# The order of the three matmuls of a split product in a float32r attention and two-MLP kernel

## The chip, the cores and the metric

The kernel runs on one core of one Trainium2 chip. The metric is the device time of one execution in microseconds, and three runs were made of the kernel before: 2424.06, 2426.97 and 2427.41 us, a median of 2426.97 us. Durations below come from one profiled execution of the same kernel, whose span, from its first instruction to its last, is 2422.0 us.

## The reference

```python
# q, k, v: (2, 6016, 256) float32; tau: scalar
qn = q / (norm(q, axis=1) + 1e-6);  kn = k / (norm(k, axis=1) + 1e-6)
a = softmax(kn.transpose(0, 2, 1) @ qn / tau, axis=-1)        # 256 x 256 for each batch
x = (v @ a).reshape(12032, 256)
x = (sigmoid(x @ w_gate) * (x @ w_val)) @ w_out               # w_gate, w_val: 256 x 1536
h = x @ w2_in                                                 # w2_in: 256 x 2048
out = (h - tanh(h)) @ w2_out                                  # 12032 x 256
```

## The kernel before

Attention is over channels, so its matrix is only 256 x 256 for each of the two batches. The kernel first streams q and k in and accumulates their product in plain float32 (`gram_chunk`, line 767), and sums squares on ScalarE and VectorE beside it. It makes the softmax, turns it (`turn_att`, line 787) and folds it into the weights: `fold` multiplies the attention matrix by `w_gate` and `w_val`, 512 columns at a time, so that v can be fed to the first MLP directly. There are 12 folds, 6 for each batch.

From there on the work goes in 32 tiles of T = 376 rows of v, 16 tiles for each batch. A tile has two stages. In the first, `U(j)` multiplies the turned v by a block of 128 columns of the gate and of the val weights, for j = 0 to 11, and `D(t, j)` multiplies the gated product by a block of `w_out` into the two banks `x2_acc`. In the second, `P_(t, i)` multiplies that result by a block of 128 columns of `w2_in`, for i = 0 to 15, and `O(t, i)` multiplies h - tanh(h) by a block of `w2_out` into `acc`. TensorE works through one hand-written order (`body`): U runs three blocks ahead of D, P_ four blocks ahead of O, and some blocks of the next tile's U are mixed into the seam between the tiles. ScalarE takes sigmoid or tanh of a finished bank and rounds the product to its high half, VectorE multiplies and makes the low half. All engines are tied by counting semaphores. TensorE waits for `g_lo_made` ahead of a D or an O, for `prod_made` ahead of a U or a P_ (its bank must be free), and for `x2_lo_made` or `acc_read_dve` ahead of a tile's first P_ or U.

Apart from the gram matrix, every product is made of halves. Each float32 operand is held as two float32r tensors, `_hi` (rounded) and `_lo` (the rest), and a product is the sum of three matmuls, high by low, low by high and high by high; low by low is left out. All of these come out of the helper `product3`, whose matmul stands on line 740. `pe.matmul(psum, a, b)` has `a` as the stationary operand (128 x 128, loaded into the array) and `b` as the moving one (376 columns in U, D and P_, 256 in O, 512 in a fold). The trace writes a matmul as output<-moving,stationary, and shows for each matmul a LDWEIGHTS of its own on the row PEld. The stationary operand is the weights in U, D and P_, the activations `g2` in O, and the turned attention in a fold. In O it has 128 columns twice and then 120, since 376 rows are 128 + 128 + 120. In the trace `x_hi`/`x_lo` are the `x2` pair, `g_hi`/`g_lo` the `g1` or `g2` pair, `x_acc` the banks `x2_acc`.

A tile has 12 x 12 matmuls in U, 12 x 6 in D, 16 x 6 in P_ and 16 x 9 in O, which is 456. Over 32 tiles these are 9984 matmuls of 376 columns and 4608 of 256. The folds add 144 of 512 columns. Divided by three that is 3328, 1536 and 48 groups, 4912 in all. No wait and no semaphore stands inside a group: the callers put their waits ahead of it, and the increment is attached to the last matmul that `product3` returns.

Of the kernel before, what the change touches and what calls it, by code (L numbers as in the profile page):

```python
# [7 lines left out]
def attn_two_mlp_kernel(  # L8
# [105 lines left out]
    with ExitStack() as ctx:  # L114
# [620 lines left out]
        def _(pe):  # L735
            def product3(psum, w, x, start, stop, shared_bank=False):

                (w_hi, w_lo), (x_hi_, x_lo_) = w, x
                for n, (a, b) in enumerate(((w_hi, x_lo_), (w_lo, x_hi_), (w_hi, x_hi_))):
                    mm = pe.matmul(psum, a, b, start=start and n == 0, stop=stop and n == 2,  # L740
                                   skip_group_check=shared_bank)
                return mm
# [48 lines left out]
            def fold(b, n, psums):  # L791

                _, w_hi, w_lo = pieces[n]
                for h in range(KC):
                    for kc in range(KC):
                        mm = product3(psums[h][:, :], both(ATT_T, ALL, kc, cols(h)),
                                      (w_hi[:, kc, :], w_lo[:, kc, :]), kc == 0, kc == KC - 1)
                mm.then_inc(fold_made, 1)

            def U(j):  # L800

                for n, w in enumerate((GATE, VAL)):
                    for kc in range(KC):
                        mm = product3(up[2 * (j % 2) + n][:, 0:T], both(w, ALL, kc, cols(j % J1)),
                                      both(VT, ALL, kc, ALL), kc == 0, kc == KC - 1)
                mm.then_inc(up_made, 1)

            def D(t, j):
                pe.wait_ge(g_lo_made, t * PER_TILE + j + 1)
                for h in range(KC):  # L810
                    mm = product3(x2_acc[h][:, 0:T], both(WOUT, ALL, j, cols(h)),
                                  both(G1, ALL, j % SLOTS, ALL), j == 0, j == J1 - 1)
                    if j == J1 - 1 and h == 0:
                        mm.then_inc(x2_half_made, 1)
                mm.then_inc(down_made, 1)
# [139 lines left out]
```

## Time and profile before

| | |
|---|---|
| median of three runs | 2426.97 us (2424.06 to 2427.41) |
| span of the profiled execution | 2422.0 us |
| TensorE matmul busy | 2391.3 us, 99%, 15132 instructions |
| TensorE weight load busy | 2366.7 us, 98%, 15132 instructions |
| VectorE busy | 1205.0 us, 50% |
| ScalarE busy | 1030.4 us, 43% |
| share of `product3` (line 740) on the chain that ended last | 94% |

Matmuls are pipelined, and the recorded duration of one overlaps the next. The time that a matmul takes out of the span is therefore read from start to start of neighbouring rows in the timeline, and not from its duration. Starts are given to 0.01 us, so the interval is taken over a stretch of rows.

### The profile page before, as it was taken

The numbers are of one execution on the slowest core, as the hardware profiler recorded it, in microseconds if no ns is written. First come the engines' busy times: TensorE is split into PE (matmuls) and PEld (weight loads), VectorE is DVE, ScalarE is ACT, GpSimd is POOL, SyncE is SP. The second block draws the span as 40 slices with busy tenths as digits, with TensorE's granted clock in tenths as the row PEclk, the third lists the DMA queues.
The fourth block names the chain that finished last, engine by engine and source line by source line (L and its number), as shares of the span: only waits on it lengthen the run. The fifth ranks groups of instructions, "written<-read, shape, count | busy, mean of one in ns | idle before, by whom it ended". The sixth has DMA issues, their size and how long they took to land.

```text
span 2422.0 us, 39823 instructions
## 1 busy us (share of the span) xinstructions
PE 2391.3 (99%) x15132; PEld 2366.7 (98%) x15132; DVE 1205.0 (50%) x2115; ACT 1030.4 (43%) x2062; POOL 105.8 (4%) x76
## 2 busy tenths in 40 slices
PE   8999999999999999999999999999999999999999
PEld 6789999999999999999989999999999999999999
DVE  6874444444444444444554444544444454444444
ACT  5543444444344444434433444444344444434443
POOL 3540000000000000000120000000000000000000
PEclk9999999999999999999999999999999999999999
DMA  9620000000000000000010000000000000000000
GB/s 309 216 68 14 7 13 7 13 13 13 13 6 13 7 13 13 13 13 7 21 33 14 13 7 13 7 13 13 13 13 6 13 7 13 13 13 11 9 6 7
DMA packets 128450, 62.08 MB, mean 26 GB/s; under 512 B 104992, under 2 KB 117280, under 8 KB 128416
## 3 DMA queue, kind: packets, MB, share of 16 engines
q1 hardware_dynamic: 125104, 49.56, 7.8%
q0 software_dynamic: 3312, 12.06, 1.5%
q8 instruction: 22, 0.36, 0.1%
q14 instruction: 12, 0.10, 0.0%
HBM read 49.28 MB, written 12.32 MB: 25 GB/s over the span
## 4 chain that ended last, share of the span: by engine, by line
PE 95%; DVE 2%; issue 1%; ACT 1%; SPq 1%; DMA 1%; DVEq 0%; ACTq 0%
PE up L740 55%; PE acc L740 22%; PE x_acc L740 17%; PE x_acc L767 1%; DVE sq_sum L529 1%; DMA qk_in<-in_k 1%; DVE g_lo L644 0%; SPq L303 0%; DVE vt_lo L621 0%; ACT squares L391 0%; SPq L287 0%; DVE norm L562 0%; DVE product L635 0%; ACT g_hi L442 0%; DVE norm L567 0%
## 5 line engine op out<-in xcount | busy, mean ns | idle before, releaser
L434 ACT ACTIVATE func_out<-up 128x376 f32<-128x376 f32 x896 | 433.5, 484 | 679.6 <-PE up L740 664.6
L644 DVE TENSOR_TENSOR g_lo<-product,g_hi 128x376 fp32r<-128x376 f32 x896 | 502.5, 561 | 433.8 <-ACT g_hi L442 429.6
L442 ACT ACTIVATE g_hi<-product 128x376 fp32r<-128x376 f32 x896 | 463.0, 517 | 491.9 <-DVE product L638 266.1
L635 DVE TENSOR_TENSOR product<-up,func_out 128x376 f32<-128x376 f32 x384 | 210.7, 549 | 485.3 <-ACT func_out L434 485.2
L740 PE MATMUL acc<-out_w_hi,g_lo 128*128 128x256 f32 (+1 forms) x1536 | 431.2, 281 | 0.0
L740 PE MATMUL acc<-out_w_lo,g_hi 128*128 128x256 f32 (+1 forms) x1536 | 430.5, 280 | 0.0
L740 PE MATMUL acc<-out_w_hi,g_hi 128*128 128x256 f32 (+1 forms) x1536 | 430.1, 280 | 0.0
L638 DVE TENSOR_TENSOR product<-up,func_out 128x376 f32<-128x376 f32 x512 | 280.8, 548 | 138.4 <-ACT func_out L434 126.0
L740 PE MATMUL up<-x_lo,in_w_hi 128*128 128x376 f32 x1024 | 341.6, 334 | 1.0 <-DVE x_lo L627 1.0
L740 PE MATMUL up<-x_hi,in_w_hi 128*128 128x376 f32 x1024 | 341.2, 333 | 0.0
L740 PE MATMUL up<-x_hi,in_w_lo 128*128 128x376 f32 x1024 | 340.0, 332 | 0.0
L740 PEld LDWEIGHTS acc<-out_w_hi,g_lo 128*128 128x128 f32 (+1 forms) x1536 | 286.0, 186 | 0.0
L740 PEld LDWEIGHTS acc<-out_w_lo,g_hi 128*128 128x128 f32 (+1 forms) x1536 | 285.8, 186 | 0.0
L740 PEld LDWEIGHTS acc<-out_w_hi,g_hi 128*128 128x128 f32 (+1 forms) x1536 | 285.7, 186 | 0.0
L740 PE MATMUL up<-vt_lo,gate_w_hi 128*128 128x376 f32 x768 | 257.0, 335 | 6.0 <-DVE product L635 3.9
L740 PE MATMUL x_acc<-g_lo,out_w_hi 128*128 128x376 f32 x768 | 257.5, 335 | 5.1 <-DVE g_lo L644 5.1
L740 PE MATMUL up<-vt_hi,gate_w_hi 128*128 128x376 f32 x768 | 257.5, 335 | 0.0
L740 PE MATMUL x_acc<-g_hi,out_w_hi 128*128 128x376 f32 x768 | 257.5, 335 | 0.0
L740 PE MATMUL up<-vt_hi,val_w_hi 128*128 128x376 f32 x768 | 257.1, 335 | 0.0
L740 PE MATMUL up<-vt_hi,gate_w_lo 128*128 128x376 f32 x768 | 256.8, 334 | 0.0
L740 PE MATMUL up<-vt_hi,val_w_lo 128*128 128x376 f32 x768 | 256.6, 334 | 0.0
L740 PE MATMUL x_acc<-g_hi,out_w_lo 128*128 128x376 f32 x768 | 256.4, 334 | 0.0
(111 smaller groups left out, 2899.9 us busy)
## 6 DMA issues: line engine op xcount, KB each, us to landing
v_in<-in_v SPq DMA_DIRECT2D x248, 48.0 KB, 2.0
qk_in<-in_q SPq DMA_DIRECT2D x29, 384.0 KB, 4.2
qk_in<-in_k SPq DMA_DIRECT2D x29, 384.0 KB, 5.3
out_rows<-out_sb SPq DMA_DIRECT2D x32, 256.0 KB, 2.2
out_rows<-out_sb SPq DMA_DIRECT2D x32, 120.0 KB, 2.2
w_stage<-in_moe_w_out POOLq DMA_DIRECT2D x7, 512.0 KB, 4.2
w_stage<-in_moe_w_gate POOLq DMA_DIRECT2D x6, 512.0 KB, 4.3
w_stage<-in_moe_w_val POOLq DMA_DIRECT2D x6, 512.0 KB, 5.4
```

The source lines that it names most:

```text
L434: act.activation(func_out[:, half, :], src[:, 0:T], func).then_inc(func_made, 1)
L442: act.activation(hi[:, i % SLOTS, :], product[:, half, :], ACT.Copy).then_inc(g_hi_made, 1)
L529: dve.tensor_tensor(sq_sum[:, which, 0:size, :], sq_sum[:, which, 0:size, :], squares[:, which, 0:size, :], ALU.add).then_inc(sq_added, 1)
L635: dve.tensor_tensor(product[:, half, :], up[2 * (i % 2) + 1][:, 0:T], func_out[:, half, :], ALU.mult).then_inc(prod_made, 1)
L638: dve.tensor_tensor(product[:, half, :], up[i % 4][:, 0:T], func_out[:, half, :], ALU.subtract).then_inc(prod_made, 1)
L644: dve.tensor_tensor(lo[:, i % SLOTS, :], product[:, half, :], hi[:, i % SLOTS, :].bitcast(F32), ALU.subtract).then_inc(g_lo_made, 1)
L740: mm = pe.matmul(psum, a, b, start=start and n == 0, stop=stop and n == 2, skip_group_check=shared_bank)
L767: mm = pe.matmul(gram[b][:, h * C:(h + 1) * C], qk_in[:, buf, 1, s, cols(h)], qk_in[:, buf, 0, s, :], start=first and s == 0 and h == 0, s ...
```

## The change

The three matmuls of a group are issued in another order. Before they were (high stationary, low moving), (low, high), (high, high); after they are (low stationary, high moving), (high, high), (high, low). The flags that open and close an accumulation stay with the first and the last of the group.

```diff
@@ -736,7 +736,7 @@
             def product3(psum, w, x, start, stop, shared_bank=False):
 
                 (w_hi, w_lo), (x_hi_, x_lo_) = w, x
-                for n, (a, b) in enumerate(((w_hi, x_lo_), (w_lo, x_hi_), (w_hi, x_hi_))):
+                for n, (a, b) in enumerate(((w_lo, x_hi_), (w_hi, x_hi_), (w_hi, x_lo_))):
                     mm = pe.matmul(psum, a, b, start=start and n == 0, stop=stop and n == 2,
                                    skip_group_check=shared_bank)
                 return mm
```

## Rows read from the trace of the kernel before

**Rows 1.** The page: busy time, share of the span and instructions of each engine
```profile
PE 2391.3 (99%) x15132; PEld 2366.7 (98%) x15132; DVE 1205.0 (50%) x2115; ACT 1030.4 (43%) x2062; POOL 105.8 (4%) x76
```

**Rows 2.** The page: chain that ended last, share of the span by engine
```profile
PE 95%; DVE 2%; issue 1%; ACT 1%; SPq 1%; DMA 1%; DVEq 0%; ACTq 0%
```

**Rows 3.** The waits of PE: who waited for whom, us in total, times, longest
```profile
PE x_acc L767 <- DMA qk_in<-in_k: 9.6, 7, 3.5
PE x_acc L740 <- DVE g_lo L644: 5.1, 1, 5.1
PE up L740 <- DVE product L635: 3.9, 2, 3.4
```

**Rows 4.** Stretches of the span: length, busy us (instructions) of each engine, clock, DMA, GB/s
```profile
400.00:800.00 400.00, 400.00 (x2590) 400.00 (x2590) 186.67 (x346) 166.14 (x340) 0.00 (x0) 1.00 0.05 11
```

**Rows 5.** Timeline of U and D: start us, us, engine, line, operation, out<-moving,stationary
```profile
1299.99 0.34 PE L740 MATMUL x_acc<-g_hi,out_w_hi 128*128 128x376 f32 x1
...
1303.09 0.33 PE L740 MATMUL x_acc<-g_hi,out_w_hi 128*128 128x376 f32 x1
```

**Rows 6.** Timeline of P_, then of O, stationary of 128 and of 120 columns
```profile
249.70 0.34 PE L740 MATMUL up<-x_lo,in_w_hi 128*128 128x376 f32 x1
...
251.24 0.28 PE L740 MATMUL acc<-out_w_lo,g_hi 128*128 128x256 f32 x1
...
251.94 0.28 PE L740 MATMUL acc<-out_w_lo,g_hi 128*120 128x256 f32 x1
...
252.30 0.33 PE L740 MATMUL up<-x_lo,in_w_hi 128*128 128x376 f32 x1
```

**Rows 7.** Timeline of a fold, PE: first matmul after a wait, then the stream
```profile
1242.20 0.50 PE L740 MATMUL x_acc<-gate_w_lo,att_t_hi 128*128 128x512 f32 x1 [0.23 <-DVE att_t_lo L599]
1242.53 0.40 PE L740 MATMUL x_acc<-gate_w_hi,att_t_lo 128*128 128x512 f32 x1
1242.77 0.39 PE L740 MATMUL x_acc<-gate_w_hi,att_t_hi 128*128 128x512 f32 x1
...
1244.81 0.39 PE L740 MATMUL x_acc<-gate_w_hi,att_t_hi 128*128 128x512 f32 x1
```

**Rows 8.** Timeline of the same fold, weight loads alone
```profile
1242.20 0.19 PEld L740 LDWEIGHTS x_acc<-gate_w_lo,att_t_hi 128*128 128x128 f32 x1 [0.54 <-DVE att_t_lo L599]
1242.31 0.19 PEld L740 LDWEIGHTS x_acc<-gate_w_hi,att_t_lo 128*128 128x128 f32 x1
1242.54 0.19 PEld L740 LDWEIGHTS x_acc<-gate_w_hi,att_t_hi 128*128 128x128 f32 x1
```

**Rows 9.** Timeline of U, matmuls and weight loads together
```profile
1306.87 0.33 PE L740 MATMUL up<-vt_lo,gate_w_hi 128*128 128x376 f32 x1
1306.87 0.19 PEld L740 LDWEIGHTS up<-vt_hi,gate_w_lo 128*128 128x128 f32 x1
1307.04 0.34 PE L740 MATMUL up<-vt_hi,gate_w_lo 128*128 128x376 f32 x1
1307.04 0.19 PEld L740 LDWEIGHTS up<-vt_hi,gate_w_hi 128*128 128x128 f32 x1
1307.22 0.33 PE L740 MATMUL up<-vt_hi,gate_w_hi 128*128 128x376 f32 x1
```

## Prediction

> **What bounds the kernel now.** I read the busy shares first, then the chain that ended last, then what TensorE waited for, and last the timeline of each stage. TensorE is busy for 99% of the span, VectorE for half and ScalarE for 43% [rows 1]. Busy shares of a pipelined engine overlap, so the chain decides, and it runs through TensorE for 95% of the span [rows 2]. TensorE's own waits are few: the longest entries are 9.6 us for the loads of q and k, 5.1 us once for a low half of g and 3.9 us for two products [rows 3]. Between 400 and 800 us the matmul row has no gap at all, the granted clock is 1.00, the 2.4 GHz level, and VectorE is busy for 187 of 400 us [rows 4]. So the time is the number of matmuls by their interval, and no other engine is near. Whatever the change brings, it brings through the interval of the 14736 matmuls of `product3`, or it brings nothing.
>
> **The intervals.** In U and D 18 intervals lie between the first and the last row shown: (1303.09 - 1299.99) / 18 = 172.2 ns [rows 5]. In P_ nine intervals of 376 columns take 251.24 - 249.70 = 1.54 us, 171.1 ns each; in O nine intervals of 256 columns take 252.30 - 251.24 = 1.06 us, 117.8 ns each [rows 6]. In a fold nine intervals of 512 columns take 1244.81 - 1242.77 = 2.04 us, 226.7 ns each [rows 7]. At 2.4 GHz, one column a cycle, the columns alone would take 156.7, 106.7 and 213.3 ns. What is over is 15.5 ns in U and D, 14.4 in P_, 11.1 in O and 13.3 in a fold: a nearly fixed cost for each pair of load and matmul. The sum over `product3` is 6912 x 172.2 + 3072 x 171.1 + 4608 x 117.8 + 144 x 226.7 ns = 1190.2 + 525.6 + 542.8 + 32.6 = 2291.2 us of the span of 2422.0 us. The other 130.8 us are the float32 gram matrix, the softmax and the waits, and the change touches none of them.
>
> **The change, part by part.** It removes no instruction that the source names and adds none. Each of the 4912 groups has the same three matmuls with the same columns. No wait stands inside a group, and the callers wait for the low half ahead of the whole group, so nothing can start sooner because the low moving operand is now used last; those edits cost nothing, and the 5.1 and 3.9 us of waits [rows 3] stay where they are. The increment stays on the third matmul, so the readers ScalarE and VectorE get the bank at the same time as before, if the three intervals together are the same. SP's and POOL's queues are not passed by anything.
>
> What is new is that the third matmul needs the stationary operand that the second one has. Whether its LDWEIGHTS goes away is the whole question, and the trace of before can't show it: nowhere in it do two neighbours have the same stationary operand. What it does show is one load for each matmul, 15132 of both [rows 1], as the helper calls `matmul` each time and nothing in the change tells it to leave a load out. I take it that the load stays, 15132 after as before. The source asks for it with every call, and no row shows a load left out.
>
> If the load stays, what is it worth that its content is already in the array? Loads lie beside work: the load for the next matmul starts in the moment in which the running one starts, 1306.87 and 1307.04 us [rows 9]. Its own length can be read where nothing covers it, at the start of a fold: the next load starts 0.11 us after the first [rows 8]. Both 172 ns and 117.8 ns cover 110 ns. Nor does a shorter load shorten the interval: with 120 stationary columns three matmuls of O take 252.30 - 251.94 = 0.36 us, 120 ns each, against 0.70 us / 6 = 116.7 ns with 128 [rows 6]. So the length of the load is hidden, and only a fixed cost of exchanging the operand, if it is part of the 11 to 15 ns, is on the path. An engine that carries out the load pays that cost, whatever was in the array. I take 0, between -68 us (worked out below, all of it gone) and +11 us, the operand bound below.
>
> **The order itself.** The same shape costs 172.2 ns in U and D and 171.1 ns in P_ [rows 5, 6]. The two differ in their tiles and banks, so placement of operands is worth about 1.1 ns. After the change the pairs of operand streamed and operand loaded beside it are the same kinds as before: before, low beside low, high beside high, and high beside the next group's high; after, high beside high twice, and low beside the next group's low. I see no reason for a sign and take 0; the bound is 9984 x 1.1 ns = 11 us to either side.
>
> The sum: the span stays at 2422.0 us. The runs' median lies 5.0 us over the profiled span, from outside the span and from spread, and that stays too. Forecast 2427 us.
>
> **A rule beside the trace.** A load takes 110 ns here and starts with the matmul ahead of it [rows 8, 9]. The Trainium skill, "TensorE: Matmul & The Clock Gate", section "LDWEIGHTS (loading the stationary operand)", gives its columns over 1.2 GHz, an estimate of 107 ns, and the trace agrees. The same page, under "Step-by-step: what each phase is for", says that loads are pulled ahead of matmuls in flight if they go to a background buffer, and that is the rule that speaks against a gain here: by it the sum stays at 2427 us. Its section "Back-to-back issue gap" gives an isolated matmul N/2.4 + 2.5 ns, 159.2 ns for 376 columns; no row here shows a matmul without a load. By that rule, if the third load were gone, one in three of the intervals would fall by 13.0, 11.9, 8.6 and 10.8 ns, 2304 x 13.0 + 1024 x 11.9 + 1536 x 8.6 + 48 x 10.8 = 56 us, an estimate of 2371 us.
>
> **Rival 1: the repeated load is left out,** by whatever turns the program into instructions or by the engine. For it speaks that every interval has 11 to 15 ns over its columns, at three sizes. Against it, that the trace has exactly as many loads as matmuls. Its price at most is the whole excess for one matmul in three: 2304 x 15.5 + 1024 x 14.4 + 1536 x 11.1 + 48 x 13.3 ns = 35.7 + 14.7 + 17.0 + 0.6 = 68 us, so 2359 us; if only half of the excess belongs to the load, 2393 us. VectorE's half share leaves room for it [rows 4]. Chance 0.10.
>
> **Rival 2: a load of the operand that is in use is not hidden.** It ends on the slow side. The place is between the second and the third matmul of a group: the load of the high half repeats what the running matmul works with, and could be held until that one has gone through. The price of an uncovered load is read at the start of a fold, where matmul two follows matmul one after 0.33 us, against 227 ns in the stream: about 100 ns [rows 7]. Fully uncovered it gives 4912 x 0.1 = 491 us, 2918 us. It decides from 1 ns a group on, 4.9 us or 0.2%. Against it: the moving operand is already the same for two neighbours, the high half in the second and third matmul, and shows no stall [rows 9]. A repeated moving operand says little of a repeated stationary one, though. Chance 0.02.
>
> **Rival 3: the order moves the interval a little.** Mechanism and price as worked out above: up to 1.1 ns on the 9984 matmuls of 376 columns, 2416 to 2438 us; it decides from 0.5 ns on. What speaks for it is that two stages of one shape differ; against it, that the kinds of pairs are the same. Chance 0.05 on the fast side beyond 0.2% and 0.07 on the slow side, the latter more because the seam between groups now has the low load of the next group beside it, with a new bank at times.
>
> **How the numbers follow.** The forecast, no change beyond 0.2%, gets what is left: 0.76. About 0.2% (4.9 us) is what a measurement of this kernel can tell from no change; the three runs of before span 3.4 us. Faster: 0.10 + 0.05 = 0.15. Slower: 0.02 + 0.07 = 0.09. The range takes in the forecast and rival 3 on both sides, 0.88 together, and leaves out rivals 1 and 2, 0.12. With the 11 us bound and the spread of the runs it is 2414 to 2439 us.
>
> **What would show it.** Count loads first: 15132 if I am right, 15132 - 4912 = 10220 if rival 1 holds by way of the program. Then the intervals of U, P_, O and a fold again: 172, 171, 118 and 227 ns by the forecast; by rival 1 the third start of a group would be followed, or preceded, by an interval near 157 ns; by rival 2 the interval from the second to the third matmul would be long, up to 270 ns. With equal counts but intervals down by some ns, the engine would find the exchange of an equal operand cheaper, and my step from a hidden load to no gain would be the wrong one. If the medians differ by over 0.2% with all intervals the same, the difference would have to lie in the waits [rows 3].

## The result and the profile after

The changed kernel takes 2433.59 us, the median of seven runs (2431.28 to 2435.59); beside them the kernel before took 2427.14 us, also the median of seven (2424.06 to 2430.48). The ratio is 1.0027, with a 95% interval from 1.0017 to 1.0038. It is slower by 0.27%, 6.5 us, a little more than the 0.2% that was taken as the limit of what can be told.

The page of the kernel after, its busy times, to be read beside [rows 1]:

```profile
span 2431.8 us, 39823 instructions
## 1 busy us (share of the span) xinstructions
PE 2394.9 (98%) x15132; PEld 2371.7 (98%) x15132; DVE 1208.0 (50%) x2115; ACT 1030.4 (42%) x2062; POOL 104.3 (4%) x76
...
## 4 chain that ended last, share of the span: by engine, by line
PE 94%; DVE 2%; issue 1%; DMA 1%; ACT 1%; SPq 0%; ACTq 0%; DVEq 0%
```

All 15132 loads are still there, and the chain runs through TensorE as in [rows 2]. The repeated load lies beside the running matmul like any other. Here is a group of P_ in which that can be seen:

```profile
249.93 0.33 PE L740 MATMUL up<-x_hi,in_w_lo 128*128 128x376 f32 x1
...
250.10 0.33 PE L740 MATMUL up<-x_hi,in_w_hi 128*128 128x376 f32 x1
250.10 0.19 PEld L740 LDWEIGHTS up<-x_lo,in_w_hi 128*128 128x128 f32 x1
250.27 0.34 PE L740 MATMUL up<-x_lo,in_w_hi 128*128 128x376 f32 x1
```

The second and the third matmul both have `in_w_hi` as the stationary operand. The third one's load starts at 250.10 us with the second matmul, and the third matmul follows 0.17 us later. The waits of PE after, the longest of them, in the columns of [rows 3]:

```profile
PE acc L776 <- DVE expd L549: 11.3, 1, 11.3
PE x_acc L767 <- DMA qk_in<-in_k: 7.5, 6, 3.8
PE x_acc L740 <- DVE g_lo L644: 5.1, 1, 5.1
PE up L740 <- DVE product L635: 3.9, 2, 3.4
```

Waits of `product3` are as before, 5.1 and 3.9 us. The 11.3 us are a wait that ends at 65 us, in the head of the kernel, ahead of the first fold, so before any matmul of `product3`; it is 3.0 to 12.9 us long in the kernels of this study, 3.7 us in the kernel before. The stretch of [rows 4] after:

```profile
400.00:800.00 400.00, 400.00 (x2590) 400.00 (x2589) 186.47 (x346) 166.53 (x341) 0.00 (x0) 1.00 0.05 11
```

No gap, the same clock. A window cut at round numbers is too coarse for 0.3%: it holds 2590 matmuls again, because it starts at another point of the tile. What shows it is the length of a tile, read from the same matmul in different tiles. The first matmul of P_ in the second and in the fourteenth tile, 12 tiles apart, in the timeline of the kernel before:

```profile
246.11 0.33 PE L740 MATMUL up<-x_lo,in_w_hi 128*128 128x376 f32 x1
...
1092.75 0.33 PE L740 MATMUL up<-x_lo,in_w_hi 128*128 128x376 f32 x1
```

and in that of the kernel after:

```profile
249.93 0.33 PE L740 MATMUL up<-x_hi,in_w_lo 128*128 128x376 f32 x1
...
255.11 0.28 PE L740 MATMUL acc<-out_w_hi,g_lo 128*128 128x256 f32 x1
...
1098.88 0.33 PE L740 MATMUL up<-x_hi,in_w_lo 128*128 128x376 f32 x1
```

A tile took 846.64 / 12 = 70.55 us and takes 848.95 / 12 = 70.75 us, 0.19 us more. Usual tiles of one execution (all but the last and the two at the change of batch) differ from one another by 0.01 us at most, the rounding of the starts, so this number is far sharper than the time of a run. Times 32 tiles it is 6.2 us, all but 0.3 us of the 6.5 us between the medians. The profiled spans differ by 9.8 us; of this 3.6 us lie before the first P_ matmul of the kernel (175.56 and 179.18 us), in the head. They are there before the new order has done anything. This is the first matmul of the first fold, which is the first of `product3`, before and then after:

```profile
95.05 0.50 PE L740 MATMUL up<-gate_w_lo,att_t_hi 128*128 128x512 f32 x1 [1.01 <-DVE att_t_lo L599]
```

```profile
98.92 0.50 PE L740 MATMUL up<-gate_w_hi,att_t_lo 128*128 128x512 f32 x1 [1.02 <-DVE att_t_lo L599]
```

No matmul in the new order comes before these. From there to the first matmul of U (125.96 and 129.84 us) it is 30.9 us in both, so the stretch of the folds is as long as before. The head's 3.6 us arise in a part of the kernel that the change doesn't touch. That part varies: the first fold starts between 93.81 and 100.35 us in the profiles of this study.

The stages inside the tile, as the mean interval from one start to the next over all matmuls of a stage in the trace (intervals over 1.2 times the usual one left out, some 3060 of P_ and 2290 to 4607 of the others kept), in ns:

| stage | before | after | difference | matmuls a tile |
|---|---|---|---|---|
| U | 172.2 | 171.7 | -0.5 | 144 |
| D | 172.0 | 171.4 | -0.7 | 72 |
| P_ | 170.9 | 172.9 | +2.1 | 96 |
| O | 117.9 | 118.6 | +0.7 | 144 |

With unrounded values 96 x 2.07 + 144 x 0.67 - 144 x 0.45 - 72 x 0.68 ns = 0.18 us of the 0.19. P_ adds 0.20 us and O 0.10 us to a tile, and U and D give 0.11 us of it back. In the rows above, the first 30 intervals of P_ take 255.11 - 249.93 = 5.18 us, where before 251.24 [rows 6] - 246.11 = 5.13 us. So it is one instruction stream with all counts equal, and its stages move by small amounts of either sign.

A stage's mean hides more than it shows. Number the 456 matmuls of a usual tile by their place in it, and take the mean interval at each place over 27 tiles of the trace before: at 376 columns these go from 165 to 178 ns, at 256 columns from 112 to 125 ns, and at every place all 27 tiles agree to 1 ns. It is no noise but a fixed pattern, and the new order is another pattern.

### The profile page after: what moved, and what is told of

Its sections match the earlier page's. It is cut to its first block, busy times and chain, and to the rows that moved or that the text cites. A ratio compares the mean times of both kernels' runs of the same rounds, so it can differ in the third digit from the quotient of the medians.

```text
span 2431.8 us, 39823 instructions
## 1 busy us (share of the span) xinstructions
PE 2394.9 (98%) x15132; PEld 2371.7 (98%) x15132; DVE 1208.0 (50%) x2115; ACT 1030.4 (42%) x2062; POOL 104.3 (4%) x76
## 4 chain that ended last, share of the span: by engine, by line
PE 94%; DVE 2%; issue 1%; DMA 1%; ACT 1%; SPq 0%; ACTq 0%; DVEq 0%
PE up L740 55%; PE acc L740 22%; PE x_acc L740 17%; DMA qk_in<-in_k 1%; PE x_acc L767 1%; DVE sq_sum L529 1%; DVE g_lo L644 0%; ACT squares L391 0%; DVE vt_lo L621 0%; SPq L287 0%; DVE norm L562 0%; DVE product L635 0%; ACT g_hi L442 0%; DVE norm L567 0%; DVE norm L566 0%
## 5 line engine op out<-in xcount | busy, mean ns | idle before, releaser
L740 PE MATMUL up<-vt_lo,val_w_hi 128*128 128x376 f32 x768 | 256.7, 334 | 0.0
```

## The experiments

Four accounts were held against each other: that the order sets the interval of a stage through the addresses of what is streamed and loaded (called the theory of place below); that a repeated stationary operand is worth something; that TensorE meets ScalarE and VectorE in memory; and that the values in the array count. The helper was given a stage name, so that the order could be chosen for each stage:

```diff
-            def product3(psum, w, x, start, stop, shared_bank=False):
+            ORDER = {'P': ('LH', 'HH', 'HL')}
+            def product3(psum, w, x, start, stop, shared_bank=False, stage="F"):
...
-                for n, (a, b) in enumerate(((w_hi, x_lo_), (w_lo, x_hi_), (w_hi, x_hi_))):
+                pairs = {"HL": (w_hi, x_lo_), "LH": (w_lo, x_hi_), "HH": (w_hi, x_hi_)}
+                for n, (a, b) in enumerate(pairs[name] for name in ORDER.get(stage, ('HL', 'LH', 'HH'))):
```

Names give the stationary half first: HL is high stationary by low moving. The order of before is HL LH HH, the changed one LH HH HL. The diffs of the orders are against the kernel before.

Only P_ alone, U and D alone, and the order by stage were run often enough (8 to 12 executions) to compare times. The others ran once: 2426.77 and 2428.54 us with x2 moved (old and new order), 2424.40 us with x2 moved by a multiple of 2048, 2426.42 us with ScalarE later, 2421.23 us with the zeros, and 2427.16 (HH HL LH), 2427.80 (HL HH LH), 2427.43 (LH HL HH) and 2427.85 us (HH LH HL). The kernel before took 2425.52 and 2428.71 us in single executions beside them. These times tell nothing at this size; what is read from these experiments is the tile, start to start.

**The new order in P_ alone** (the diff above).

> The new order in P_ alone, all other stages as before. Both profiles repeat to 0.01 us from tile to tile: 70.55 us before, 70.75 us after, and between starts of neighbouring matmuls P_ went from 170.9 to 172.9 ns, U from 172.2 to 171.7, D from 172.0 to 171.3, O from 117.8 to 118.4. Theory (the order sets the interval of each stage by itself): P_ near 172.9 ns, the others as before, a usual tile of 70.75 us, about 6 us over before, ratio 1.002 to 1.003. Rival (the interval of a stage hangs on what its neighbours do, or the change of a whole tile has one cause that the order in P_ alone does not carry): P_ stays near 170.9 ns, the tile near 70.55 us, ratio 1.000. Rival that the difference comes from the head of the kernel: ratio 1.000, since the folds are as before.

Measured: 2429.97 us against 2425.43 us, ratio 1.0020 (1.0010 to 1.0029). The same two matmuls, 12 tiles apart:

```profile
248.14 0.33 PE L743 MATMUL up<-x_hi,in_w_lo 128*128 128x376 f32 x1
...
1096.22 0.33 PE L743 MATMUL up<-x_hi,in_w_lo 128*128 128x376 f32 x1
```

A tile of 70.67 us. P_ took 172.6 ns, U 172.2 and D 172.0 as before. The tile fell short of the 70.75 us expected, since P_ rose by 1.7 and not by 2.1 ns, and since O, whose order was not touched, fell from 117.9 to 117.6 ns. P_ and O alternate in the stream, and what stands beside a matmul counts too. The new order in P_ alone costs 0.12 us a tile, part of the 0.19.

**The new order in U and D alone.**

```diff
+            ORDER = {'U': ('LH', 'HH', 'HL'), 'D': ('LH', 'HH', 'HL')}
```

> The new order in U and D alone; P_, O and the folds as before. Theory (each stage by itself): U near 171.7 and D near 171.3 ns, so a tile gains 144 x 0.45 + 72 x 0.7 ns = 0.11 us, 70.44 us, about 3.6 us in all, ratio 0.9985, faster than both kernels. Rival (intervals hang on the neighbours or on chance of the execution): U and D as before at 172.2 and 172.0 ns, ratio 1.000 or above.

Measured: 2422.80 us against 2425.43 us, ratio 0.9987 (0.9979 to 0.9996). Twelve tiles:

```profile
245.46 0.33 PE L743 MATMUL up<-x_lo,in_w_hi 128*128 128x376 f32 x1
...
1090.50 0.33 PE L743 MATMUL up<-x_lo,in_w_hi 128*128 128x376 f32 x1
```

70.42 us a tile, 0.13 less than before; U 171.7, D 171.1, P_ 170.9, O 117.9 ns. As expected, this part of the change is a small gain.

The two runs together say something about O. The new order in P_ adds 0.12 us a tile and in U and D it takes 0.13 us off, so these three stages alone would leave the tile as it was. Yet the changed kernel's tile is 0.19 us longer. The other 0.2 us, about 6.6 us in 32 tiles and as much as the whole measured loss, come only when O has the new order beside them: O goes from 117.6 ns with the order changed in P_ alone to 118.6 ns, P_ from 172.6 to 172.9 ns. The new order in O alone was not run, so how much of this is O's own and how much its meeting with P_ stays open.

**x2 at another address, old order.** P_ streams x2. It was moved behind all other tensors, and a dummy holds its old place:

```diff
-        x2_hi, x2_lo = pair("x2", [P, KC, T])
+        x2_gap = sb("x2_gap", [P, 2, KC, T])
...
         out_sb = sb("out_sb", [P, len(SUBS), C])
+        x2_pad = sb("x2_pad", [P, 72])
+        x2_hi, x2_lo = pair("x2", [P, KC, T])
```

> The order of before, with the two halves of x2, which P_ streams, at another place of SBUF (45472 bytes a partition further on, 416 beyond a multiple of 2048). No other tensor moves. Theory of place (the interval depends on where the streamed and the loaded operand lie): P_ moves away from 170.9 ns by more than 0.3 ns, in either direction, and U and O stay at 172.2 and 117.8. Rival (values in the array, or the order as such): P_ stays within 0.2 ns of 170.9, tile 70.55 us.

```profile
243.77 0.34 PE L742 MATMUL up<-x_lo,in_w_hi 128*128 128x376 f32 x1
...
248.93 0.28 PE L742 MATMUL acc<-out_w_lo,g_hi 128*128 128x256 f32 x1
...
1092.41 0.34 PE L742 MATMUL up<-x_lo,in_w_hi 128*128 128x376 f32 x1
```

A tile of 70.72 us, almost what the changed order costs, with nothing changed in the order. P_ went to 171.7 ns, U stayed near its 172.2 (172.3) and D at 172.0. O was expected to stay at 117.8 and went to 118.3: again the neighbour of P_ moved with it.

**x2 at that other address, new order.** The same diff on the changed kernel.

> The new order everywhere, with x2 at the same other place as in the run before this one. Theory of place: P_ moves away from 172.9 ns, and the difference between the two orders in P_, 2.1 ns at the old place, is another one here, perhaps of the other sign. Rival (the order as such costs 2.1 ns in P_): P_ stays 2.1 ns over the run with the old order at this place.

```profile
249.00 0.34 PE L742 MATMUL up<-x_hi,in_w_lo 128*128 128x376 f32 x1
...
254.14 0.28 PE L742 MATMUL acc<-out_w_hi,g_lo 128*128 128x256 f32 x1
...
1096.36 0.34 PE L742 MATMUL up<-x_hi,in_w_lo 128*128 128x376 f32 x1
```

70.61 us a tile, P_ at 171.5 ns. At this address the new order is the better one, by 0.11 us a tile, and P_ costs 0.2 ns less with it instead of 2.1 more. U and D gain as they did at the old address, and O is slower by 0.4 ns. The first 30 intervals of P_ take 5.14 us here and 5.16 with the old order, against 5.18 and 5.13 at the old address. The loss of the changed kernel is not a property of the order; it is the order together with where the tensors lie.

**x2 moved by a multiple of 2048 bytes, old order.** The output rows' tensor and a dummy fill the old place.

```diff
-        x2_hi, x2_lo = pair("x2", [P, KC, T])
+        out_sb = sb("out_sb", [P, len(SUBS), C])
+        x2_gap = sb("x2_gap", [P, 736])
...
-        out_sb = sb("out_sb", [P, len(SUBS), C])
+        x2_pad = sb("x2_pad", [P, 224])
+        x2_hi, x2_lo = pair("x2", [P, KC, T])
```

> The order of before, with x2 moved by 43008 bytes a partition, 21 times 2048, where the earlier move was 22 times 2048 and 416 more. The tensor of the output rows, which TensorE doesn't touch, takes part of the old place; nothing else moves. In both traces the intervals of U and P_ inside a tile repeat with every fourth block of 128 weight columns, that is every 2048 bytes. Theory (the address counts by its remainder to 2048): P_ 170.9 ns and a tile of 70.55 us, as before. Rival (any other address changes it, or a coarser bank than 2048 bytes counts): P_ moves by 0.3 ns or more and the tile leaves 70.55 us by more than 0.03.

```profile
245.70 0.33 PE L742 MATMUL up<-x_lo,in_w_hi 128*128 128x376 f32 x1
...
1092.34 0.33 PE L742 MATMUL up<-x_lo,in_w_hi 128*128 128x376 f32 x1
```

846.64 us for 12 tiles, to the last digit as before, and each of the 456 places of a tile has its old interval to within 0.1 ns. A move about as long as the one above, with remainder 0 instead of 416 bytes, changes nothing. So it is not the move that counts; the two moves fit the remainder of the address to 2048 bytes, or to a divisor of it. No third address was tried.

**ScalarE's and VectorE's work later, old order.**

```diff
...
+                if not isinstance(n, int) or n > 1:
+                    act.wait_ge(extra_made, n - 1)
+                act.activation(extra[:, :], src[:, 0:T], func).then_inc(extra_made, 1)
                 act.activation(func_out[:, half, :], src[:, 0:T], func).then_inc(func_made, 1)
```

> The order of before. ScalarE applies sigmoid or tanh to each finished bank twice, the first time into a tensor that nothing reads, so that everything ScalarE and VectorE do in the tiles comes about 0.48 us later against TensorE's matmuls, and there is half as much again for ScalarE to do. No operand of TensorE moves. Theory (the interval is set by TensorE's own two reads, streamed operand and loaded operand, by where they lie): U 172.2, D 172.0, P_ 170.9, O 117.8 ns and a tile of 70.55 us, as before. Rival (the intervals come from TensorE's meeting with ScalarE and VectorE in SBUF or PSUM): they move by 0.3 ns or more, the tile by 0.1 us or more.

The page's busy times and the twelve tiles:

```profile
PE 2389.7 (99%) x15132; PEld 2365.6 (98%) x15132; DVE 1211.1 (50%) x2115; ACT 1330.4 (55%) x2958; POOL 105.1 (4%) x76
```

```profile
247.51 0.33 PE L746 MATMUL up<-x_lo,in_w_hi 128*128 128x376 f32 x1
...
1094.15 0.33 PE L746 MATMUL up<-x_lo,in_w_hi 128*128 128x376 f32 x1
```

846.64 us again, with 300 us more of ScalarE. That is less than the half as much again that was expected, and the shift is not an even 0.48 us either: in a usual tile, the products come 0.4 us later in most places and up to 1.2 us in some, the halves of vt hardly at all. Even so, each of the 456 places has its old interval to within 0.1 ns. Had TensorE's meeting with the others in memory set the pattern, it would have moved where they moved; it is ruled out as the cause.

**Zeros in the array.** The low half of `w2_in` is made as high minus high.

```diff
-                pool.tensor_tensor(lo, staged(n), hi.bitcast(F32), ALU.subtract).then_inc(w_split, 1)
+                rest_of = hi.bitcast(F32) if SECOND_BLOCK <= n < SECOND_BLOCK + 2 * J2 * P // WCOLS else staged(n)
+                pool.tensor_tensor(lo, rest_of, hi.bitcast(F32), ALU.subtract).then_inc(w_split, 1)
```

> The order of before, with zeros in place of the low half of w2_in: the instruction that splits the weights subtracts the high half from itself. This leaves out the high x times low w part of the first product of the second MLP. One in three of P_'s matmuls then has an array of zeros. Theory of place: P_ 170.9 ns, tile 70.55 us as before. Rival (the values in the array set the interval): P_ moves by 0.3 ns or more, most of all the interval of the matmuls with the low weights.

Twelve tiles lie between 243.67 and 1090.31 us, 846.64 us once more, and every place as before to within 0.1 ns. Zeros in a third of P_'s loads change nothing. (The run's 2421.23 us against 2425.52 us are not a gain: its tiles are equal, and its head was short, the first P_ at 173.12 us.)

**All other orders, everywhere.** The four left, each as `ORDER`'s default.

> All groups in the order high-high, high-low, low-high (stationary, moving). The first two have the same stationary operand, as two of the three have in the new order, but at another place of the group, and no neighbours have the same moving operand. Theory (a repeated stationary operand is worth nothing, intervals follow the addresses of neighbours in the stream): each stage within 1.5% of before, the second matmul's load still there, 15132 loads, and no interval that stands out where the stationary operand repeats; tile between 70.3 and 70.9 us. Rival (what the new order saves in U and D, 0.5 and 0.7 ns, is the repeated operand): U and D near 171.7 and 171.3 ns again.

> All groups in the order high-low, high-high, low-high: the first two have the same stationary operand, the last two the same moving one. It is the new order read backwards. Theory of neighbours and places: a tile between 70.3 and 70.9 us, with stages up and down independently. Rival (repeated stationary operand helps U and D, costs P_): U near 171.7, D near 171.3, P_ near 172.9 ns, as in the new order.

> All groups in the order low-high, high-low, high-high: the last two have the same stationary operand, no two the same moving one. So far U and D took 172.2 and 172.0 ns in the two orders that begin with high-low (before, and high-low, high-high, low-high) and 171.6 to 171.7 and 171.2 to 171.3 in the two that begin otherwise. If the first matmul of a group decides, U and D are near 171.7 and 171.3 here; if it is the cyclic sense of the three, in which this order differs from before, the change and high-high, high-low, low-high, they are near 172.2 and 172.0. By neither is a repeated stationary operand worth anything: 15132 loads, tile between 70.3 and 70.9 us.

> All groups in the order high-high, low-high, high-low: no neighbours in a group have the same stationary operand, the first two the same moving one. If the first matmul of a group decides, U and D are near 171.6 and 171.2 ns, although nothing repeats in the array: that would show finally that their gain with the changed order is not the repeated operand. If the repeated operand is what gains there, 172.2 and 172.0.

Measured, mean intervals in ns and the tile in us:

| order | repeated in the group | U | D | P_ | O | tile |
|---|---|---|---|---|---|---|
| HL LH HH (before) | moving | 172.2 | 172.0 | 170.9 | 117.9 | 70.55 |
| LH HH HL (after) | both | 171.7 | 171.4 | 172.9 | 118.6 | 70.75 |
| HH HL LH | stationary | 171.6 | 171.2 | 171.4 | 118.2 | 70.51 |
| HL HH LH | both | 172.2 | 172.0 | 171.4 | 118.4 | 70.67 |
| LH HL HH | stationary | 171.8 | 171.1 | 171.4 | 118.7 | 70.61 |
| HH LH HL | moving | 171.6 | 171.2 | 172.8 | 117.7 | 70.58 |

Each has its 15132 loads. U and D are cheap in the four orders that don't begin with HL, and dear in the two that do. The last row decides about the repeated stationary operand: no two neighbours of a group share one there, and U and D have the gain all the same; the order HL HH LH has one and lacks it. The page of HH LH HL, for the loads:

```profile
PE 2387.7 (98%) x15132; PEld 2363.4 (97%) x15132; DVE 1210.7 (50%) x2115; ACT 1030.3 (42%) x2062; POOL 104.8 (4%) x76
```

In P_ another feature sorts them: 172.8 and 172.9 ns where HL comes last, 170.9 for the order of before, 171.4 for the rest. The theory had left open which feature would count, and the cyclic sense, one of its two guesses for U and D, fell with LH HL HH.

**An order for each stage.**

```diff
+            ORDER = {'U': ('HH', 'HL', 'LH'), 'D': ('HH', 'HL', 'LH'), 'O': ('HH', 'LH', 'HL')}
```

> The best order so far for each stage: high-high, high-low, low-high in U and D (171.6 and 171.2 ns where all groups had it), the order of before in P_ (170.9 ns, the lowest of all six orders), and high-high, low-high, high-low in O (117.7 ns where all groups had it, against 117.9 before, but beside a P_ that was slower). Theory (stages are separable, only O and P_, which alternate, touch each other): U 171.6, D 171.2, P_ 170.9, O 117.7 to 118.2, so a tile is 70.55 - 144 x 0.6 - 72 x 0.8 ns = 70.41 us with O as before, 70.37 to 70.45 us with its bounds; 3 to 6 us under before in all, ratio 0.998 to 0.999. Rival (O's low value came from its slower neighbour P_, as with the order changed in P_ alone, where O fell to 117.6 with its own order untouched): O or P_ rises by 0.5 ns or more and the tile is at or over 70.42 us, what the new order in U and D alone reached.

Measured: 2421.67 us against 2427.31 us, ratio 0.9972 (0.9962 to 0.9983), where 0.998 to 0.999 was expected; the quotient of the two medians is 0.9977. It is faster than the kernel before. The changed kernel was not run beside it, but its tile is 0.35 us longer.

```profile
248.18 0.33 PE L743 MATMUL up<-x_lo,in_w_hi 128*128 128x376 f32 x1
...
1092.90 0.33 PE L743 MATMUL up<-x_lo,in_w_hi 128*128 128x376 f32 x1
```

70.39 us a tile: U 171.5, D 171.2, P_ 170.9 and O 117.9 ns. U and D kept their gain. O did not: 117.7 ns had come from the company of a slower P_, as the rival said, but neither stage rose and the tile is below 70.42 us, so the rival's result didn't come. Times 32 the tile gives 5.1 us, beside 5.6 us between the medians.

## Why the prediction was right or wrong

**What bounds the kernel, and the form of the sum: right.** The time is the number of matmuls by their interval. Of the 6.5 us between the medians 6.2 us are the difference of the tile, and in a tile no wait, no count and no clock changed.

**The load stays: right.** 15132 loads in all six orders.

**A load whose content is in the array already saves nothing: right, and now shown.** In the changed kernel the interval from the second to the third matmul, ahead of which the operand repeats, and the one from the first to the second, ahead of which it doesn't, are 172.3 and 172.5 ns in P_, 171.9 and 172.0 in U, 172.0 and 170.7 in D, 118.8 and 119.0 in O (means over 27 usual tiles). HH LH HL has no repeated operand in its groups and is as fast in U and D as the changed order, which has one. So of the 11 to 15 ns of excess nothing came back by repeating that the other differences of 1 or 2 ns wouldn't cover, and rival 1 fell, the estimate of 2371 us by the isolated interval with it. The Trainium skill, "TensorE: Matmul & The Clock Gate", section "Step-by-step: what each phase is for", with its loads pulled ahead in the background, is on the side of what was measured: the repeated load starts with the matmul ahead of it, 250.10 us for both.

**The repeated load is hidden: right.** Rival 2 wanted an interval of up to 270 ns; the longest of all places in the changed kernel's tile is 179 ns.

**The order itself, "I take 0", bound 11 us: this step was wrong, in its value and in how its bound was made.** The argument was that the kinds of pairs, low beside low and high beside high, are the same before and after. The kinds don't set the interval: with x2 at another address and the same order, so the same kinds, P_ went from 172.9 to 171.5 ns. In P_ the order works together with x2's address, and P_ moved by 2.1 ns, twice the bound of 1.1 ns taken from the difference between two stages. O was left out of that bound altogether and moved by 0.7 ns. In us, P_ added 6.4 and O 3.0, and U and D took 3.7 off. That the measured 2433.59 us lies in the range of 2414 to 2439 us, in the case that had been given a chance of 0.07, is therefore luck in part: had U and D moved as P_ did, the 9984 matmuls alone would have cost 21 us. The forecast of no change beyond 0.2%, with 0.76, was missed by a little. A better working would have looked at single places of a tile in the trace of before. They go from 165 to 178 ns at the same shape, which says that something moves the interval by several ns where the loads and columns are equal, and that 1.1 ns, a difference between two means, is no bound for what a new order can do.

**The median over the profiled span, "5.0 us, and that stays too": it didn't, and it did no harm.** It is 1.8 us after. In every execution whose own span is recorded, the time is 1.7 to 1.9 us over it; the rest of the 5.0 us was that the profiled execution of before was a short one. The forecast of a median by a median, 2427 us, doesn't hang on it. Whether the new order in the folds shifts the head is answered by the traces above: the stretch of the folds takes the same 30.9 us, and the head differs before they begin.

**What stays open.** The experiments show that x2's address decides about P_'s interval together with the order, that 416 bytes beyond a multiple of 2048 and a multiple of 2048 differ, and they rule out the other engines, and zeros against other values in P_'s low weights. They don't show which access meets which: the streamed and the loaded operand are the near guess, since the intervals at the places of a tile repeat with every fourth block of 128 columns in U and P_, 2048 bytes of weights; but the banks and slots repeat with four blocks as well, and the weights themselves were not moved. Nor was a smaller divisor of 2048 tried. That U, D and O also follow addresses is argued from P_ and not shown, and the share of O's own new order in the loss is open.

## What to carry to other kernels

Putting equal stationary operands next to each other was worth nothing here, where each matmul still carries its own load and the load is hidden under the matmul before; look at the count of loads first. With TensorE never idle, the order of accumulating matmuls and the place of their operands in SBUF were still worth two to three tenths of a per cent, by stage and with either sign. So choose the order for each stage by a run, and expect that a later shift of an address can change the answer. To see effects of this size, compare the length of a loop iteration between two traces, start to start, and not the times of single runs. And don't take stages to be independent: the new order in P_ alone and in U and D alone add up to nothing here, and the whole change, O with it, lost 0.19 us a tile.

## What the runs showed of the hardware that was not expected

A usual tile of 456 matmuls repeats to within 0.01 us of 70.55, over the usual tiles of an execution, with 300 us more work on ScalarE and with zeros for a third of P_'s stationary operands. Inside it the single intervals are a fixed pattern, from 165 to 178 ns at 376 columns, and in these two runs and in the one with x2 moved by a multiple of 2048 bytes each of the 456 came back to within 0.1 ns. Moving one streamed tensor by 45472 bytes raised it to 70.72 us, moving it by 43008 bytes, 21 times 2048, left it at 70.55 us. The six orders of three independent matmuls gave 70.51 to 70.75 us. And a stage's interval depends on its neighbours in the stream: O, untouched, went from 117.9 to 117.6 ns when P_ changed its order, and to 118.3 ns when P_'s operand moved.
